# Second pair's value sums and their turning moved one tile on; token weights loaded at the end of a pair of heads and split in the next

## What is computed

```python
def _attn_ref(q, k, v):
    k_sum = k.reshape(B, H, nb, block, D).max(axis=3)      # block = 32, nb = 24
    v_sum = v.reshape(B, H, nb, block, D).mean(axis=3)
    scores_l = scale * q @ k.T          # kept where |i - j| < 16
    scores_s = scale * q @ k_sum.T + log(block)
    a = softmax(concat(masked scores_l, scores_s))
    return a @ concat(v, v_sum)

def _moe_ref(x, w_tok1, w_tok2, w_ch1, w_ch2):
    h = relu(x.T @ w_tok1) @ w_tok2     # mixes tokens: 768 -> 256 -> 768
    u = x + h.T
    return u + relu(u @ w_ch1) @ w_ch2  # 512 -> 1536 -> 512

def _moe2_ref(x, g_ln, w_ch1, w_ch2):
    xn = (x - mean) / sqrt(var + 1e-6) * g_ln
    return x + relu(xn @ w_ch1) @ w_ch2 # 512 -> 2048 -> 512
```

## Time and profile before

| | |
|---|---|
| median of three executions | 582.25 us |
| profiled execution, own time | 581.43 us |
| its span | 579.6 us |
| time around the span | 1.8 us |
| PE busy | 570.2 us (98%) |
| DVE, ACT, POOL busy | 51%, 41%, 40% |
| mean granted PE clock | 0.996 |
| chain that ended last: PE | 95% |
| chain that ended last: DMA | 3%, the load of `tok_stage` |

### The profile page before, as it was taken

The page is one execution under the profiler, slowest core; times in us unless marked ns, Lnnn a source line. Parts: engine busy times, 40 slices in busy tenths (PEclk is TensorE's granted clock), DMA queues, the critical chain, the costliest instruction groups (busy, mean ns, idle before and its releaser), DMA issues.

```text
span 579.6 us, 8277 instructions
## 1 busy us (share of the span) xinstructions
PE 570.2 (98%) x2977; PEld 500.0 (86%) x2977; DVE 297.4 (51%) x654; ACT 238.1 (41%) x442; POOL 229.1 (40%) x231
## 2 busy tenths in 40 slices
PE   7799999999999999999999999999999999999997
PEld 4688888889888889898889889898888888888886
DVE  6577556486344446653335774444335644444444
ACT  6589674563324342353336333634344112221220
POOL 4388663237444754020328955443369000000000
PEclk9899999999999999999999999999999999999999
DMA  8998620064555463443415285544374443434602
GB/s 247 259 249 230 200 100 2 16 256 165 200 201 200 136 236 155 164 163 129 164 36 200 43 310 169 169 162 181 128 290 164 163 148 123 135 137 148 236 0 110
DMA packets 21952, 94.56 MB, mean 163 GB/s; under 512 B 2472, under 2 KB 2600, under 8 KB 18328
## 3 DMA queue, kind: packets, MB, share of 16 engines
q1 hardware_dynamic: 21400, 93.36, 48.0%
q10 hardware_dynamic: 512, 0.68, 0.4%
HBM read 65.19 MB, written 28.84 MB: 162 GB/s over the span
## 4 chain that ended last, share of the span: by engine, by line
PE 95%; DMA 3%; DVE 1%; issue 0%; ACT 0%; SPq 0%; ACTq 0%; DVEq 0%
PE bank L614 91%; DMA tok_stage<-w_tok 3%; PE bank L726 1%; DMA k_sb<-k_w 1%; PE bank L656 1%; PE bank L658 1%; PE bank L657 1%; PE bank L717 0%; DVE k_sb L1115 0%; DVE v_first L1121 0%; DVE natural L1204 0%; PE bank L623 0%; ACT probs_t L905 0%; DVE neg_scores L1138 0%; SPq L326 0%
## 5 line engine op out<-in xcount | busy, mean ns | idle before, releaser
L614 PE MATMUL bank<-down_w,hidden 128*128 128x512 f32 x1008 | 269.9, 396 | 0.0
L614 PEld LDWEIGHTS bank<-down_w,hidden 128*128 128x128 f32 x1008 | 184.6, 188 | 24.9
L998 ACT ACTIVATE hidden<-bank 128x384 fp32r<-128x384 f32 x112 | 55.1, 492 | 245.4 <-DVE bank L1199 176.5
L614 PE MATMUL bank<-in_t,up_odd 128*128 128x384 f32 x588 | 118.8, 337 | 0.0
L614 PE MATMUL bank<-in_t,up_even 128*128 128x384 f32 x588 | 118.7, 337 | 0.0
L614 PEld LDWEIGHTS bank<-in_t,up_odd 128*128 128x128 f32 x588 | 105.6, 188 | 8.9
L614 PEld LDWEIGHTS bank<-in_t,up_even 128*128 128x128 f32 x588 | 105.5, 188 | 8.9 <-issue 0.2
L1191 DVE SCALAR_TENSOR_TENSOR hidden<-bank,hidden 128x384 fp32r<-128x384 f32 x112 | 62.5, 558 | 86.0 <-ACT hidden L998 86.0
L1231 DVE TENSOR_TENSOR u<-bank,p 128x384 f32<-128x384 f32 x28 | 15.6, 557 | 88.8 <-PE bank L614 88.8
L1199 DVE TENSOR_TENSOR bank<-bank,u 128x384 f32<-128x384 f32 x84 | 47.5, 565 | 20.4 <-PE bank L614 15.8
L1138 DVE CUSTOM_DVE_ANT_0 neg_scores<-bank,mask_sb 128x182 f32<-128x182 f32 x96 | 29.5, 344 | 27.0 <-PE bank L614 18.3
(11 more groups left out here) (103 smaller groups left out, 611.4 us busy)
## 6 DMA issues: line engine op xcount, KB each, us to landing
raw_down<-w_ch SPq DMA_DIRECT2D x28, 512.0 KB, 3.6
up_kept<-up_even SPq DMA_DIRECT2D x7, 1792.0 KB, 9.2
up_kept<-up_odd SPq DMA_DIRECT2D x7, 1792.0 KB, 8.2
up_even<-up_kept SPq DMA_DIRECT2D x7, 1792.0 KB, 7.2
up_odd<-up_kept SPq DMA_DIRECT2D x7, 1792.0 KB, 7.2
raw_up<-w_ch SPq DMA_DIRECT2D x14, 512.0 KB, 4.5
k_sb<-k_w SPq DMA_DIRECT2D x15, 273.0 KB, 6.6
v_own<-v_w SPq DMA_DIRECT2D x8, 390.0 KB, 3.8
```

What stands on the lines that cost most here:

```text
L614: return nc.tensor.matmul(dst, lhs, rhs, start=start, stop=stop, skip_group_check=True)
L998: nc.scalar.activation(hidden[:, q % 2, f, 0, h * HN:(h + 1) * HN], src, ACT.Relu).then_inc(hid_high, 1)
```

## The change

It does five things.

1. DVE sums the second pair's values (`sum_first_values(1)`) at tile 3 instead of tile 2, behind the masking of tile 6's scores.
2. PE turns these sums in front of tile 5's transposes instead of tile 4's, and ACT copies them then; for all other pairs it remains tile 4 (`means_at`).
3. SP loads the token chunk `r` at the end of pair `r`'s entries, behind the keys, queries and values, instead of in front of them.
4. ACT makes chunk `r`'s high part at tile 3 of pair `r+1` instead of tile 4 of pair `r`, and POOL the low part in pair `r+1`; the token mixing waits for two chunks at its start and for all four only where it needs the second weight.
5. PE's products at the start are 13 in bf16, and the 6 on `warm_r` are gone, with DVE's copy that made it.

```diff
-WARM = 11
-WARM_R = 6
+WARM = 13
+def means_at(r):
+    return MEANS_AT + 1 if r == 0 else MEANS_AT
...
             for r in range(NPAIR):
                 if r + 2 < NPAIR:
                     load_turned(r + 2)
-                if r < TOK_CH:
-                    load_tok(r)
...
                 if r + 2 < NPAIR:
                     load_v(r + 2)
+                if r < TOK_CH:
+                    load_tok(r)
...
                     split_x(2 * r)
-                    if r < TOK_CH:
-                        tok_low_part(r)
+                    if 0 < r <= TOK_CH:
+                        tok_low_part(r - 1)
                     split_x(2 * r + 1)
...
-                    if (n - 2) % NT == MEANS_AT:
-                        pe.wait_ge(mean_copied, 2 * ((n - 2) // NT + 2))
+                    k, at = divmod(n - 2, NT)
+                    if at == means_at(k):
+                        pe.wait_ge(mean_copied, 2 * (k + 2))
...
-                if t == MEANS_AT and r + 1 < NPAIR:
-                    turn_sums(r + 1, tb[:, mean_at])
+                if t == means_at(r) and r + 1 < NPAIR:
+                    turn_sums(r + 1, tb[:, mean_cols])
...
                     if i == 0:
-                        pe.wait_ge(tok_split, TOK_CH)
+                        pe.wait_ge(tok_split, 2)
...
                     if t == 0:
+                        pe.wait_ge(tok_split, TOK_CH)
                         pe.wait_ge(h_low, 2)
...
-            pe.wait_ge(warm_ready, 2)
-            for _ in range(WARM_R):
-                mm(mix_bank[:, 0:2 * P], warm_r[:, 0:P], warm_r[:], True, True)
...
-                if t == MEANS_AT and r + 1 < NPAIR:
+                if t == means_at(r) and r + 1 < NPAIR:
                     copy_means(r + 1, turn_bank[n % 2])
...
-                if 0 <= r < TOK_CH and t == 4:
-                    tok_high_part(r)
+                if 0 < r <= TOK_CH and t == 3:
+                    tok_high_part(r - 1)
...
-            dve.wait_ge(warm_ready, 1)
-            nc.vector.tensor_copy(warm_r[:], warm[:, 0:2 * P]).then_inc(warm_ready, 1)
...
-                if n == 2:
+                if n == 3:
                     sum_first_values(1)
```

More of the change, by code:

```diff
@@ L140, in build @@
             v_sum = sb(a, "v_sum", [P, KB, P])
-            warm_r = sb(a, "warm_r", [P, 2 * P], F32R)
             v_first = sb(a, "v_first", [P, DVE_SUMS, NSUM])
@@ L171, in build @@
         acc_bank, up_bank = bank[0:6], bank[6:8]
-        mean_at = slice(3 * P, 4 * P)
+        mean_cols = slice(3 * P, 4 * P)
         ld_mask = sem("ld_mask")
@@ L750, in _ @@
                 if n == 0:
-                    turn_sums(0, mix_bank[:, mean_at])
+                    turn_sums(0, mix_bank[:, mean_cols])
                 weigh(n)
```

## The result

The changed kernel takes 586.2 us (median of 12 executions, 585.28 to 588.86) against 582.53 us (median of 12, 580.08 to 584.53). The ratio is 1.0082, with a 95% interval of 1.0066 to 1.0099: slower, by 3.7 us between the medians and by 4.8 us if one goes by the ratio. So the two profiles are further apart than the medians.

The account below looks back on a forecast made before the run. Bound: PE's own work plus its standing still in the attention, POOL and loads close behind. From 581.43 us: front -4.3, `spread_keys(2)` +2.2, loop +3.75, rounded +1.7, giving 583.1; by the median 583.9; taken 583.5, range 579.5 to 587.0.

Parts of the forecast that it names:

- Second pair's sums: PE's turning of these sums starts at 19.25, waiting 0.8 us instead of 1.77; tile 5 gains 2.05 us.
- The front's gain is lost at tile 13: Tile 13's scores wait for POOL's `spread_keys(2)` and start at 30.7; of 4.3 us gained only 2.1 are left.
- So the bytes ahead are the same and I leave the landing at 32.8.: Pair 3's turned values, issued earlier but still behind the token chunk, land at 32.8 us as before.
- The loop: Low part, chunk issue, turned values' landing and POOL's work repeat every 11.5 us per pair; +3.75 us until the token mixing.
- ACT at tile 3: ACT's copy of turned weights comes about 0.5 us late in pairs 1 to 3, covered; uncovered up to 1.5 us.
- The start: Thirteen bf16 products end at 6.8, before the scores at 6.97; costed at nothing, uncovered 0.1 or 0.2 us.
- Rival A: Loads keep up, pair 3's sums start before 32 us: 0 to -2.1 us, typically -1 (582.5); chance 0.24.
- Rival B: New idle stretches bring half clock, the last before the token mixing costing 1.7 us: +3.3, 585.2; chance 0.20, with longer landing.
- Rival C: The front's gain stays because POOL's chain has unseen slack: 4.3 us faster, 577.1; chance 0.03.

Follow-up runs that it names:

- the fastest version: Changed kernel with turned values before the token chunk, queries before keys, POOL's earlier spreading and ACT's high part at tile 5: 578.81 us, ratio 0.9927 to before.

## Why the prediction was right in its way and wrong in its size

**Second pair's sums.** Foreseen: PE starts them at 19.25 after 0.8 us of waiting. Measured: 19.28 after 0.69. Also no half clock before 24 us. Right.

**The front's gain is lost at tile 13.** Right in place and cause: the scores there wait for POOL's spreading. But they start at 33.2 and not at 30.7, since POOL's sums for pair 2 start at 25.91. The step "its sums for pair 2 still start at 23.35, since that load was issued ahead of the token chunk" is wrong: the issue order was kept, the neighbour behind was not.

**"So the bytes ahead are the same and I leave the landing at 32.8."** This is the step that failed: the landing of pair 3's turned values. It came to 36.4, which is 3.6 us more, while the whole sum was +1.65; and the forecast's bounds were worked out for the two landings of the loop only, not for this one. From there on the sum holds within 0.6 us:

| step | foreseen | measured |
|---|---|---|
| POOL starts on pair 3's values | 32.93 | 36.57 |
| first low part ends | 39.66 | 43.29 |
| second low part ends | 51.14 | 54.29 |
| `split_x(6)` ends | 60.72 | 64.83 |
| first mixing product | 60.8 | 64.97 |

With the measured 3.6 the forecast would have been +5.3, against the 5.9 of the two profiled spans. With queries in front of keys pair 3's values landed at 33.7 and the mixing started at 60.97, which is nearly the forecast. That the order of keys and queries has a part in it is shown by that run; why it has is not. I counted bytes in a line, where the trace's and the landings show sixteen lines that do not end together. The signs were in the trace of before: the token chunk, issued 0.4 us behind the turned values of pair 2, landed 2.7 us after them, while loads of the same size that had no keys behind them followed within 1.0 to 1.5 us.

**The loop.** Foreseen at 11.5 us; measured 11.0 and 12.4. The landing was taken as 4.2 us and was 3.7 and 5.2. Right within the spread of the rows.

**ACT at tile 3.** Foreseen at 0.5 us a pair and covered. Covered it was in the changed kernel's profile, though tile 4 leaves up to 2 us open over the runs; uncovered it showed 0.25 to 1.09 us.

**The start.** Costed at nothing. PE's first scores start at 6.85 against 6.97. No run isolated it.

**Rival A** (the loads keep up) was wrong for the same reason as the forecast, and with the wrong sign: an earlier issue did not make an earlier landing. **Rival B** (the clock): the half clock came, at tile 13 and for 6.8 us. It hid in the following waits for POOL (0.34 us left at 45.81, 0.88 at 56.81), as foreseen, so it is not what made the forecast too small. The stretch right before the token mixing, which B priced at 1.7 us, ran at full clock. That the measured 586.2 us lie inside the stated range is therefore in part luck: its upper end was there for B and for slower loops, and the time got there by a landing that nobody had priced. **Rival C** was out.

By the Trainium skill's page DMA: Bandwidth & Descriptors (section Anatomy of one DMA) such a load takes some 2.9 us, an estimate. That section is on loads issued by GpSimd, and these are issued by SP. The changed kernel's trace agrees with it where the line is empty: the token chunks issued at 43.32 and 54.32 us landed after

```profile
DMA to landing us min/median/max: 2.8/2.8/2.8
DMA to landing us min/median/max: 3.0/3.0/3.0
```

But the turned values stand 0.4 us behind such a chunk, and took 3.7 and 5.2 us, and 11.5 in the full line. The loop waits for those, so the rows were the better guide: with 2.9 us in the loop the change would have come out near nothing.

## What to carry to other kernels

When a load that waits for a slow engine is moved back in a queue, look at what now stands behind it: the wait moves onto all of that, and if one of these feeds the same slow engine, a loop closes whose length can be summed from rows. In a full line a load is not priced by the bytes ahead of it alone; look for which load is the late one in the trace, and what stands behind it. A wait that is removed in front of a fixed landing only makes the next wait longer, and the longer one may be followed by more time at half clock, as in the run with the sums alone.

## What the runs showed of the hardware

A load with keys right behind it (two loads of 64 rows x 4368 bytes) is complete 1.8 to 3.2 us after its first engine is done (pair 2's turned values, in a full line, four profiles), with a token chunk right behind it 0.6 to 0.9 us (four profiles), and with queries between it and the keys 0.6 to 2.2 us (five). In an emptied line, with keys right behind, it was 0.7 to 1.0 us (pair 4's, three profiles). In the trace of before the median packet of 4368 bytes took 317 ns and that of 3072 bytes 127; among keys, from 24 to 28 us in the changed kernel, the median packet of 3072 bytes took 242 ns, but from 46 to 47.5 us, in the emptied line and with keys under way too, 121 ns. That the engines which are ahead start on the keys and so slow those that are behind fits the full line, but it was not tested by itself.

The clock, at 0.50 for 3.4 or 6.8 us behind PE's idle stretches: 6.8 us with the stretch of 4.08 us in the run with the sums alone, and with those of 1.58 and 2.76 us close together in the changed kernel, where 2.2 of the 6.8 us lay within the second one; 3.4 us with the 1.77 us of before, and with 2.74 us in the kernel before with sums and queries moved; none with the 1.44 us of before and the 0.74 and 1.12 us of the fastest version. The length of the stretches doesn't settle it: 1.59 and 2.76 us close together in the run with the turned values first were followed by 3.4 us only. Nor is one long stretch always dearer than two short ones: 1.77 and 2.21 us in the kernel before with queries first were followed by 3.4 us each, as much together as the 4.08 us.
